# Low parts of the first weights by GpSimd's adding transfers, output by channels, two moved steps on VectorE

## The reference

```python
mag = sqrt(a_re**2 + a_im**2); scale = minimum(mag, 0.999) / (mag + 1e-6)
S = complex(a_re, a_im)[t] * scale * S + outer(k[t], v[t])      # for each t: a 48 x 48 state per head
y[t] = q[t] @ S.real                                            # linear attention with complex decay
h = y @ w_in                       # 384 x 2048
g = maximum(h, 0) + log1p(exp(-abs(h)))
x = g @ w_out                      # 2048 x 384
out = (((x @ w1) * (x @ w2)) @ w3) @ w_out2      # 384 x 1024 twice, 1024 x 1024, 1024 x 384
```

## Time and profile before

| | us |
|---|---|
| median of 3 runs | 1001.27 |
| lowest, highest | 998.71, 1001.32 |
| profiled execution: device time | 1001.37 |
| profiled execution: span of the trace | 999.6 |
| PE busy in it | 908.0 |
| DVE busy in it | 608.2 |
| ACT busy in it | 428.4 |

### The profile page before, as it was taken

One profiled execution on the slowest core, in us unless ns is written; L12 is line 12 of the kernel. 1 busy time (PEld: TensorE's weight loads), 2 busy tenths in 40 slices (PEclk: granted clock), 3 DMA queues, 4 the chain that ended last, 5 costly groups with the idle time before them and its releaser, 6 DMA issues.

```text
span 999.6 us, 14524 instructions
## 1 busy us (share of the span) xinstructions
PE 908.0 (91%) x5442; PEld 827.3 (83%) x5442; DVE 608.2 (61%) x974; ACT 428.4 (43%) x618; POOL 70.3 (7%) x56
## 2 busy tenths in 40 slices
PE   0963839999999999999899999998999999999998
PEld 0533739889989889899899999998888888888887
DVE  5978878989898898899889732355221212121211
ACT  3152263575574674664664654586102020202011
POOL 0000000000000000000000000000222222222221
PEclk9995668999999999999999999999999999999999
DMA  9666066273372380570570540421101010101000
GB/s 336 234 192 187 20 189 131 74 182 102 106 175 78 121 214 25 151 193 13 154 193 13 145 106 13 148 86 46 33 1 64 1 64 1 63 0 63 0 32 32
DMA packets 98663, 99.52 MB, mean 100 GB/s; under 512 B 6944, under 2 KB 91936, under 8 KB 98592
## 3 DMA queue, kind: packets, MB, share of 16 engines
q1 hardware_dynamic: 98592, 98.59, 34.4%
HBM read 63.96 MB, written 29.88 MB: 94 GB/s over the span
## 4 chain that ended last, share of the span: by engine, by line
PE 64%; DVE 22%; DVEq 6%; issue 3%; ACT 3%; DMA 2%; ACTq 0%; SPq 0%
PE ps_p L1312 8%; PE ps_p L1314 8%; PE ps_p L1313 8%; PE ps L1312 4%; PE ps L1314 4%; PE ps L1313 4%; PE ps_ay L1348 3%; PE ps L1509 3%; PE ps L1507 3%; PE ps L1508 3%; DVE sp L1191 2%; PE ps_ay L1313 2%; PE ps_ay L1314 2%; DVE an L1018 2%; PE ps_ay L1312 2%
## 5 line engine op out<-in xcount | busy, mean ns | idle before, releaser
L646 POOL TENSOR_TENSOR abl<-ab,abh 128x512 fp32r<-128x512 f32 x48 | 69.4, 1445 | 922.5 <-DVE abh L1295 922.5
L1312 PE MATMUL ps_p<-x1h,win_h 128*128 128x384 f32 x336 | 118.3, 352 | 16.9 <-DVE sp L1191 16.9
L1312 PE MATMUL ps<-g_h,wo_h 128*128 128x384 f32 x384 | 132.7, 346 | 0.0
L1314 PE MATMUL ps<-g_h,wo_l 128*128 128x384 f32 x384 | 129.6, 337 | 0.0
L1313 PE MATMUL ps<-g_l,wo_h 128*128 128x384 f32 x384 | 129.3, 337 | 0.0
L1314 PE MATMUL ps_p<-x1h,win_l 128*128 128x384 f32 x336 | 113.9, 339 | 0.0
L1313 PE MATMUL ps_p<-x1l,win_h 128*128 128x384 f32 x336 | 113.7, 338 | 0.0
L1348 PE MATMUL ps_ay<-stq,stk 96*128 96x128 f32 x384 | 56.7, 295 | 35.8 <-DMA vt<-in_v 12.8
L1286 DVE TENSOR_TENSOR ab<-ps_ay,bc 128x512 f32<-128x512 f32 x24 | 16.6, 693 | 117.0 <-ACT bc L914 117.0
L762 ACT ACTIVATE g_h<-sp 128x768 fp32r<-128x768 f32 (+1 forms) x71 | 55.5, 781 | 74.2 <-DVE sp L1191 74.2
L1348 PEld LDWEIGHTS ps_ay<-stq,stk 96*128 96x128 f32 x384 | 54.1, 208 | 37.1 <-issue 24.0
(11 more groups left out here) (167 smaller groups left out, 2050.9 us busy)
## 6 DMA issues: line engine op xcount, KB each, us to landing
qk_scr<-tt SPq DMA_DIRECT2D x16, 576.0 KB, 4.7
stq<-qk_scr SPq DMA_DIRECT2D x48, 192.0 KB, 4.8
qk_scr<-pp SPq DMA_DIRECT2D x16, 576.0 KB, 4.2
stk<-qk_scr SPq DMA_DIRECT2D x48, 192.0 KB, 4.5
an<-in_a_re SPq DMA_DIRECT2D x8, 576.0 KB, 4.0
an<-in_a_im SPq DMA_DIRECT2D x8, 576.0 KB, 5.1
qk<-in_q SPq DMA_DIRECT2D x8, 576.0 KB, 7.7
qk<-in_k SPq DMA_DIRECT2D x8, 576.0 KB, 8.6
```

Of the source, the lines that this page charges most:

```text
L646: tensor_tensor(abl[:, m % AR, :], ab[:, m % 2, :], abh[:, m % AR, :].bitcast(F32), ALU.subtract).then_inc(ab_lo, 1)
L1312: mm(o, wh, xh, start=start, stop=False)
L1314: return mm(o, wl, xh, start=False, stop=stop)
```

## The change

Four things are changed.

1. **Low parts of w_in and w_out.** `raw_low` is gone from DVE (8 subtractions). `raw_high` on ScalarE now makes two copies of a piece: the rounded high part, and the piece times -1 rounded into the place of the low part. In the text of the change `raw_high` reads `piece(i)` both times; what the second copy leaves there is minus the high part. GpSimd then issues, for each piece, 3 or 4 transfers (one for each group of 128 rows, 28 in all, of 128x512 or 128x384 elements) that read the weights from DRAM a second time and add them to what stands in the low part's place. The raw buffers come free with `raw_hi` instead of `raw_lo`; the first `up` waits for the 28 transfers (raw_lo of 16 x 28).
2. **Output by channels.** `down2` now loads blocks of `w34h`, `w34l` and moves `abh`, `abl` of 512 columns: 3 blocks of 3 matmuls for each m instead of 4 of 3. The output is (384, 3072) in DRAM, stored in three parts of 128 channels.
3. **q in two halves.** The product `tt = q * pp` is one of 128x2304 elements before, two of 128x1152 now: the first stands behind mask 4, the second behind the sum. `store_q` waits for each half.
4. **keys behind the sum.** `prep_keys` moves from behind mask 5 to behind the sum of j = 5.

```diff
@@ load_piece, store_q (SP)
-                    wait(raw_lo, before[-1] + 1)
+                    wait(raw_hi, before[-1] + 1)
...
-                wait(prep_q, m + 1)
...
                 for i in range(2):
+                    wait(prep_q, 2 * m + i + 1)
                     eng.dma_start(c_p(qk_scr[i]), by_g(tt[:, i, :])).then_inc(q_wr, 16)
...
-            wait(raw_lo, 5)
+            wait(raw_hi, 5)
@@ gpsimd
+            for i in range(8):
+                eng.wait_ge(raw_hi, i + 1)
+                for g in range(G if i < 4 else 4):
+                    eng.dma_start(piece_to[i][1][:, g, :], piece_src[i][:, g, :].bitcast(F32R), accum_op=ALU.add)\
+                        .then_inc(raw_lo, 16)
@@ raw_high (scalar)
-                act(piece_to[i][0], piece(i), ACT.Copy).then_inc(raw_hi, 1)
+                act(piece_to[i][0], piece(i), ACT.Copy)
+                act(piece_to[i][1], piece(i), ACT.Copy, scale=-1.0).then_inc(raw_hi, 1)
...
-            eng.wait_ge(raw_lo, 8)
@@ out_tile (scalar)
-                for s_ in range(4):
-                    eng.wait_ge(o_mm, 4 * t + s_ + 1 + 4)
+                for mo in range(G):
+                    eng.wait_ge(o_mm, G * t + mo + 1 + G)
@@ vector
-            after_mask = {0: steps("run", 1), 1: steps("run", 5), 2: steps("carry", 2), 3: by[:2], 4: ["q"], 5: ["inverse", "keys"]}
-            after_sum = {0: steps("run", 2), 1: steps("run", 6), 2: steps("carry", 4), 3: by[2:3], 4: ["p2"], 5: []}
+            after_mask = {0: steps("run", 1), 1: steps("run", 5), 2: steps("carry", 2), 3: by[:2], 4: [("q", 0)], 5: ["inverse"]}
+            after_sum = {0: steps("run", 2), 1: steps("run", 6), 2: steps("carry", 4), 3: by[2:3], 4: [("q", 1), "p2"], 5: ["keys"]}
...
-            def raw_low(i):
-
-                eng.wait_ge(raw_hi, i + 1)
-                ve.tensor_tensor(piece_to[i][1], piece(i), piece_to[i][0].bitcast(F32), ALU.subtract).then_inc(raw_lo, 1)
@@ tensor
-            eng.wait_ge(raw_lo, 8)
+            eng.wait_ge(raw_lo, 16 * 28)
...
-                for s_ in range(4):
+                for mo in range(G):
                     if m == 0:
-                        eng.wait_ge(o_ev, 4 * t + s_ + 1)
-                    ts = slice(P * s_, P * (s_ + 1))
-                    ah, al = abh[:, m % AR, ts], abl[:, m % AR, ts]
-                    mm(ps_o[s_], ah, w34h[:, m, :], start=m == 0, stop=False)
-                    mm(ps_o[s_], ah, w34l[:, m, :], start=False, stop=False)
-                    last = mm(ps_o[s_], al, w34h[:, m, :], start=False, stop=m == NM2 - 1)
+                        eng.wait_ge(o_ev, G * t + mo + 1)
+                    ms = slice(P * mo, P * mo + P)
+                    last = mm3(ps_o[mo], w34h[:, m, ms], w34l[:, m, ms], abh[:, m % AR, :], abl[:, m % AR, :],
+                               m == 0, m == NM2 - 1)
```

More of the change, by code:

```diff
@@ L159, in build @@
                   ps_ay[:, 1, 0:DM], ps_k[:, 0:DM], ps_ay[:, 0, 0:DM]]
-        ps_o = [ps_2[:, 0, 0:DM], ps_2[:, 1, 0:DM], ps_2[:, 2, 0:DM],
-                ps_ay[:, 1, 0:DM]]
+        ps_o = [ps_2[:, mo, :] for mo in range(G)]
         consts = sem("consts")
@@ L612, in _ @@
                 load_x2_first()
+            out_c = out.rearrange("(g p) t -> p g t", p=P)
             def store(t, u):
-                wait(o_ev, 4 * t + 4 + 4)
-                eng.dma_start(out[bass.ts(t, T2), :].rearrange("(s p) n -> p s n", p=P),
-                              ost[:, u, :, :]).then_inc(o_wr[u], 16)
+                wait(o_ev, G * t + G + G)
+                eng.dma_start(out_c[:, :, bass.ts(t, T2)], ost[:, u, :, :]).then_inc(o_wr[u], 16)
             load_x2(1, 1)
@@ L624, in _ @@
             store(NT2 - 2, 0)
-            for s_ in range(4):
-                wait(o_ev, 4 * (NT2 - 1) + s_ + 1 + 4)
-                eng.dma_start(out[T2 * (NT2 - 1) + P * s_:T2 * (NT2 - 1) + P * s_ + P, :], ost[:, 1, s_, :]).then_inc(o_wr[1], 16)
+            for mo in range(G):
+                wait(o_ev, G * (NT2 - 1) + mo + 1 + G)
+                eng.dma_start(out_c[:, mo, bass.ts(NT2 - 1, T2)], ost[:, 1, mo, :]).then_inc(o_wr[1], 16)
             wait(o_wr[0], 16 * NT2 // 2 + 16)
-            wait(o_wr[1], 16 * NT2 // 2 + 16 + 3 * 16)
+            wait(o_wr[1], 16 * NT2 // 2 + 16 + (G - 1) * 16)
         @block.gpsimd
@@ L1075, in prep @@
                         prep_p_(m, even, first)
-                    elif piece == "q":
-                        prep_q_(m)
+                    elif piece[0] == "q":
+                        prep_q_(m, piece[1])
                     elif piece == "p2":
@@ L1151, in _ @@
             prep(0, True, ["m2"])
-            raw_low(0)
             prep(0, True, ["newton", "scale start", "scale"] + steps("a", 0, 1) + steps("run", 1, 2))
-            raw_low(1)
             prep(0, True, steps("run", 3, 4, 5, 6, 7))
-            raw_low(2)
             prep(0, True, ["ends"] + steps("carry", 1, 2, 4))
-            raw_low(3)
-            prep(0, True, steps("carry", 8, 16, 32) + by + ["p", "q", "p2", "inverse", "keys", "keys end"], first=True)
+            prep(0, True, steps("carry", 8, 16, 32) + by + ["p", ("q", 0), ("q", 1), "p2", "inverse", "keys", "keys end"], first=True)
             prep(1, False, ["m2", "newton", "scale start", "scale"] + steps("a", 0, 1))
@@ L1162, in _ @@
                 prep(1, False, steps("run", i - 3))
-                raw_low(i)
             prep(1, False, steps("run", 4))
@@ L1173, in _ @@
                 prep(1, False, between[2 * i + 1])
-                if i == 2:
-                    raw_low(7)
-            prep(1, False, ["q"])
+            prep(1, False, steps("q", 0, 1))
             x1_low(0)
```

27 lines of the change are left out of this document (14 added, 13 removed).

## The result

The changed kernel takes 1028.56 us (median of 4 runs, 1025.95 to 1032.49) against 1000.97 for the kernel before, run beside it: a ratio of 1.0284, 95 % interval 1.0247 to 1.032. The forecast was 995.3, with a range to 1013. Its sign was wrong.

A forecast was written before the change was run, and what follows sets the result against it. PE was taken as busy nearly everywhere after the start, so only the start, holes in the slots and matmul time could pay. From 1001.4: start +1.8, slots -5.8, steps 4 and 5 -2.1 gave 995.3 us, range 981.5 to 1013.

The forecast's parts named there:

- What bounds the kernel: Whole kernel: PE is mostly busy, so only a shorter start, fewer holes in the slots and cheaper matmuls pay.
- Start, DVE and ACT: Start: subtractions leave DVE, the negated copy of piece 0 costs 1.4; first `up` could start 10.4 us earlier, at 119.5.
- 75.1 + 16 R = 135.9: Start: first `up` waits for the last 16 transfers, one after another from 75.1 at 3.8 us each, until 135.9.
- The term 75.1: Start: piece 4's second copy is done at 75.1 and its transfers begin then, the first 12 having had 60 us.
- The term 16 R: Start: 16 periods of one adding transfer, 3.8 us each, twice the idle row's 1.9 because an addition reads two places: 60.8.
- One at a time: Start: GpSimd's adding transfers run singly, period 3.0 to 4.4 us, total 985 to 1004; the forecast case, chance 0.38.
- rival C: Wait of the first `up`: transfer period above 4.4 us makes the kernel slower than before, 1006.5 or 1024; chance 0.27.
- What a late `up` is worth: Start: break-even is `up` at 134.1, the full gain of 10.3 needs 123.8; at 135.9 the start loses 1.8.
- Slots: PE's holes for DVE's sum, slots 0 to 5: q in halves gains 4.8, both moves 5.8 us, bounds 0 and 8.
- Rival D: Slots: the moves do nothing, because mask or `g_low` then comes last for PE; 1001.1 us, chance 0.08.
- Steps 4 and 5: Matmuls of 512 columns gain 0.05 in each of 48 groups, 2.4, less 0.3 at the end: net 2.1 us.
- Early transfers and w3: Start: early transfers delay the w3 load by two to four us, at no cost, within about 4 us of slack.

The follow-up runs named there:

- plain transfers: The changed kernel with its 28 GpSimd transfers only writing, not adding, in the same 512 bytes, so three are in flight: 977.31 us, one run.
- without backlog: The changed kernel with pieces 0 to 3 subtracted by GpSimd in SBUF, only pieces 4 to 7 by adding transfers, one in flight: 1022.16 us.
- adding_alone: The kernel before with only the low parts by adding transfers, scratch area of 512 bytes: 1041.62 us, ratio 1.0428.
- vector_lows: The changed kernel with low parts subtracted on DVE again, one ScalarE copy and no GpSimd transfers; the other parts stay: 987.19 us, ratio 0.988.

## Why the prediction was wrong, by its steps

**What bounds the kernel**, and the three stages: right; the whole difference lies in them.

**Start, DVE and ACT**: right. The first mask was forecast at 83.4 and stood at 83.09; the full gain of the start as 10.4 us, and with plain transfers `up` came 10.8 and `down(0,0)` 10.8 us earlier. The negated copy of piece 0 was put at 1.4 and cost 0.9 against the kernel before (14.68 there, 15.62 after).

**The step that failed is the sum 75.1 + 16 R = 135.9, in both of its terms:** its start, "Pieces 0 to 3 (12 transfers from 12.4 on) have 60 us", and R = 3.8 for each of the 16. `up` came at 169.37.

**The term 75.1.** I gave R only to the last 16 and never multiplied it by the first 12. Even at the quiet 3.8 that would have been 46 us, of the 60; at the 5.6 of the busy row it is 67. It was 78.9, and the last 16 began 16 us late (91.2 for 75.1). In that stretch SP loads w3, the raw pieces, and decays, queries and keys; the page's slices (25 us each; DMA share in tenths) of before, then of after:

```profile
DMA  9666066273372380570570540421101010101000
```

```profile
DMA  9998692007536238057065171051101010101000
```

The first four slices were at 9, 6, 6 and 6 before the change: 12 transfers of 256 KB more, each alone and with its latency grown by the load, could not be quick there. I had looked at PE's and the clock's slices only.

**The term 16 R**: 3.8 was near on light queues (3.8 to 4.2), by a wrong reason: luck. An addition does not double the period: one GpSimd transfer costs 3.0 by itself, the addition 0.9 to 1.0. And R is not one number: six of the 16 lay beside loads, at 4.2 to 8.1. The mean was 4.9 (5.1 without backlog). The two errors are 16.1 us and 16 x 1.09 = 17.4: together the 33.5 between 135.9 and 169.4. This splits one trace; it doesn't say what mending one term would bring, as the kernel without backlog shows (`up` 3.8 earlier, not 16). One at a time was the right choice among the rivals, and rival C the right mechanism, with R above 4.4; but it too counted only the last 16, and at 4.9 would have had `up` at 153.5.

**What a late `up` is worth**: right. Break-even was put at `up` = 134.1; 169.4 - 134.1 = 35.3, and the start lost 35.2. `g_low(0,0)` is last, with 8.4 us, as its chain was told. In the four other kernels whose `up` was released by a transfer, `down(0,0)` came 19.6 to 20.1 us behind it, not 19.0, so the rule is good to about 1 us.

**Slots**: 5.8 forecast, 4.8 (3.2 to 6.4) measured with both moves alone; the split was wrong in q. q's halves gave 1.9 us (0.4 to 3.4), 2.3 by PE's holes, not 4.8: the holes of j = 4 did shrink by 4.7 in all, but I did not count what DVE, with the same work in all, hands on to j = 5, j = 6 and the state, 2.4 in this trace. I had used that argument for the keys and not for q. The keys gave 1.9 (0.8 to 2.9), which 1.0 fits: 1.04 in slot 5, where the hole is gone, the rest in tenths elsewhere. The 6.3 between the two traces are more than the moves: the trace of before has two falls of the granted clock in the slots, 1.1 us each (below), and the trace of after has none; 0.5 is the hole ahead of step 4. Rival D is out, as both moves together gave a gain clear of nothing.

**Steps 4 and 5**: 2.1 forecast, 4.7 in the traces, 4.3 by the runs. The mis-sized term is the 0.05 per group: I took 2.11 against 2.04 to 2.08 for `down2` alone. The 2.08 of the `up2` block behind `down2` was in the earlier trace rows, and also falls to 2.04. That makes 2.11 + 2.08 - 2.04 - 2.04 = 0.11 per group, 48 x 0.11 = 5.3, less 0.3 of the tail. (The clock falls once in this stage in both traces, so it doesn't enter.) Why the `up2` block behind `down2` was slower in the old form, no run tells.

**Early transfers and w3**: right that the slack covers them; even 6 us cost nothing.

## What to carry to other kernels

A queue's time is the sum over all its transfers, by the load of the stretch in which each lies; a backlog ahead of the ones you look at counts like their own length. Ask how many transfers may be in flight before asking how long one takes: here 512, 640 and 1536 bytes of room made 1028.6, 988.0 and 981.9 us of the same kernel. And when work is moved within a full engine, follow it to every later hand-over, not only to the hole that shrinks.

## What was not expected of the hardware

**The granted clock can fall behind a hole of about 2 us, and closing such holes can pay twice.** At j = 5 of slot 0 before the change PE stands 1.87 us idle (the twin of the 1.87 in the earlier trace rows); windows of 1 us around it (PE busy first, granted clock third from the end):

```profile
205.00:206.00 1.00, 1.00 (x12) 0.75 (x12) 0.91 (x2) 0.04 (x1) 0.00 (x0) 1.00 0.19 55
...
209.00:210.00 1.00, 1.00 (x5) 1.00 (x4) 0.84 (x2) 0.86 (x3) 0.00 (x0) 0.50 1.27 153
210.00:211.00 1.00, 1.00 (x5) 1.00 (x4) 1.00 (x2) 0.96 (x1) 0.00 (x0) 0.50 1.15 216
211.00:212.00 1.00, 1.00 (x6) 1.00 (x5) 1.00 (x1) 0.97 (x1) 0.00 (x0) 0.61 0.57 148
212.00:213.00 1.00, 1.00 (x7) 1.00 (x7) 1.00 (x1) 0.20 (x1) 0.00 (x0) 1.00 0.01 3
```

Behind the hole the clock is at 0.50 (1.2 GHz) for 3.4 us. The same group lasts 11.4 us from hole to hole in slot 0 (208.48 to 219.87) and 10.3 in slot 2 (352.00 to 362.31), where the same hole is followed by no fall: 1.1 us.

```profile
219.87 0.45 PE L1312 MATMUL ps_p<-x1h,win_h 128*128 128x384 f32 x1 [0.24 <-DVE sp L1191]
...
362.31 0.44 PE L1312 MATMUL ps_p<-x1h,win_h 128*128 128x384 f32 x1 [0.61 <-DVE sp L1191]
```

The profile of before has three falls behind holes of PE (slot 0, slot 4, and the 2.60 ahead of step 4, which costs 1.6: 303.56 against 301.9 us in the two kernels with the old output and no fall there), `adding_alone` four (three in the slots), the output by channels two (one in the slots), q in halves one behind its hole of 2.00. In the kernels with the keys moved, whose holes in the slots are at most 0.95 (1.6 at j = 4 with the keys alone), no profile shows one in the slots. This may be a part of why both moves and the output together gave 12.0 us (10.4 to 13.7) where their single results, 4.8 and 4.3, sum to 9.1, and why `vector_lows`, whose profile has no such fall, ran within 987.15 to 987.41. It is not shown: each profile is of one execution, and the intervals of the two figures overlap. Why the hole ahead of step 4, 1.9 to 2.6 us in all kernels, is followed by a fall in some executions and not in others stays open.

**A GpSimd subtraction of 3.4 us makes a two-input product of DVE that meets it 3.1 to 3.2 us longer**, while 28 adding transfers issued by GpSimd do not: DVE's products of 128x1152 stay at 1.34 to 1.36 us beside them.

**A transfer from GpSimd without addition, one at a time on light queues, takes 3.0 us from issue to issue**; a store of that size by SP takes 1.9 from issue to landing.
